# Forming the 32x32 inverses of three units by squaring on TensorE instead of column by column on VectorE

## The reference

```
for t in range(S):
    y[:, :, t] = einsum('bhd,bhde->bhe', rt, state)
    Sa = einsum('bhde,bhe->bhd', state, at)
    state = state * wt[:, :, None, :] - einsum('bhd,bhe->bhde', Sa, bt) + einsum('bhd,bhe->bhde', vt, kt)
h = x @ w_in;  x = maximum(0.01 * h, h) @ w_out            # 3072 x 320, 2048 wide
out = (sigmoid(x @ w_gate) * (x @ w_val)) @ w_out2          # 1536 wide
```

## Time and profile before

| what | value |
|---|---|
| time, median of 3 runs | 1166.05 us (1156.57 to 1169.82) |
| the profiled execution | 1176.43 us |
| its span, first to last instruction | 1174.7 us |
| TensorE busy | 1061.2 us, 90% |
| VectorE busy | 596.3 us, 51% |
| ScalarE busy | 397.6 us, 34% |
| mean granted TensorE clock | 0.956 of full |
| DMA queue of instructions (q8) | 125 packets, 2.05 MB |

### The profile page before, as it was taken

The page is one execution under the profiler, slowest core; times in us unless marked ns, Lnnn a source line. Parts: engine busy times, 40 slices in busy tenths (PEclk is TensorE's granted clock), DMA queues, the critical chain, the costliest instruction groups (busy, mean ns, idle before and its releaser), DMA issues.

```text
span 1174.7 us, 35939 instructions
## 1 busy us (share of the span) xinstructions
PE 1061.2 (90%) x15840; PEld 905.7 (77%) x15840; DVE 596.3 (51%) x1307; ACT 397.6 (34%) x782; POOL 109.4 (9%) x100
## 2 busy tenths in 40 slices
PE   3476595888999999989999999999999999999998
PEld 3476474776878787877778787888888888888887
DVE  8674674796667865666756232443323232322322
ACT  2323232333443533343344334553322222222322
POOL 7201102022020202020200000000000000000000
PEclk9996698988999998989999999999999999999999
DMA  5836215536353533444351205330010102020000
GB/s 174 260 70 217 57 29 142 130 93 172 85 139 87 165 84 107 114 131 94 105 140 51 70 8 170 102 93 23 15 45 1 59 1 59 1 59 1 23 1 23
DMA packets 134985, 99.79 MB, mean 85 GB/s; under 512 B 96560, under 2 KB 111920, under 8 KB 134832
## 3 DMA queue, kind: packets, MB, share of 16 engines
q1 hardware_dynamic: 132384, 85.06, 27.2%
q0 software_dynamic: 2448, 12.45, 3.0%
HBM read 78.61 MB, written 18.87 MB: 83 GB/s over the span
## 4 chain that ended last, share of the span: by engine, by line
PE 75%; DVE 9%; issue 8%; DMA 3%; ACT 2%; POOL 1%; SPq 1%; ACTq 0%; DVEq 0%; POOLq 0%
PE pair_low L866 12%; PE pair L919 11%; PE pair_low L919 6%; PE bank L919 6%; DVE prod L1402 3%; PE bank L939 3%; PE bank L938 3%; PE bank L937 3%; DVE t_unit L1406 2%; PE bank L840 2%; PE bank L831 2%; PE pair_low L883 2%; PE pair_low L884 1%; PE pair_low L885 1%; PE bank L883 1%
## 5 line engine op out<-in xcount | busy, mean ns | idle before, releaser
L1452 DVE TENSOR_TENSOR g_lo<-g_full,g_hi 128x512 fp32r<-128x512 f32 x168 | 122.7, 730 | 237.1 <-ACT g_hi L1167 237.0
L1167 ACT CAST g_hi<-g_full 128x512 fp32r<-128x512 f32 x168 | 104.4, 621 | 134.7 <-DVE g_full L1504 131.6
L866 PE MATMUL pair_low<-x_hi,w_up 128*128 128x512 f32 x440 | 131.8, 432 | 6.2 <-ACT x_hi L1176 3.4
L1160 ACT ACTIVATE g_full<-pair_low 128x512 f32<-128x512 f32 x88 | 52.7, 599 | 211.3 <-PE pair_low L866 198.6
L1402 DVE TENSOR_TENSOR prod<-t_unit,p_unit 128x126 f32<-128x126 f32 (+22 forms) x341 | 93.9, 275 | 24.8 <-DMA p_unit<-p_dram 14.6
L1406 DVE TENSOR_TENSOR t_unit<-t_unit,prod 128x126 f32<-128x126 f32 (+22 forms) x341 | 96.7, 284 | 11.7
L866 PEld LDWEIGHTS pair_low<-x_hi,w_up 128*128 128x128 f32 x440 | 82.3, 200 | 25.8 <-ACT x_hi L1176 3.5
L1504 DVE TENSOR_TENSOR g_full<-pair,h_sb 128x512 f32<-128x512 f32 x36 | 24.9, 691 | 112.8 <-PE pair L919 112.0
L866 PE MATMUL pair_low<-x_lo,w_up 128*128 128x512 f32 x264 | 78.4, 407 | 0.0
L1504 DVE TENSOR_TENSOR g_full<-bank,h_sb 128x512 f32<-128x512 f32 x36 | 24.9, 691 | 94.7 <-PE bank L919 86.3
L383 POOL TENSOR_TENSOR k_sb<-k_sb,inv 128x512 f32<-128x512 f32 x24 | 32.5, 1360 | 368.0 <-DMA k_sb<-in_kF 368.0
(11 more groups left out here) (232 smaller groups left out, 2564.4 us busy)
## 6 DMA issues: line engine op xcount, KB each, us to landing
b_sb<-in_bF SPq DMA_DIRECT2D x12, 512.0 KB, 6.3
a_sb<-in_aF SPq DMA_DIRECT2D x24, 256.0 KB, 6.4
k_sb<-in_kF SPq DMA_DIRECT2D x12, 512.0 KB, 5.0
v_sb<-in_vF SPq DMA_DIRECT2D x12, 512.0 KB, 6.7
r_sb<-in_rF SPq DMA_DIRECT2D x12, 512.0 KB, 8.6
p_unit<-p_dram SPq DMA_DIRECT2D x22, 256.0 KB, 4.1
w_raw<-in_wF SPq DMA_DIRECT2D x20, 260.0 KB, 3.6
stage<-in_w_out POOLq DMA_DIRECT2D x7, 640.0 KB, 7.2
```

The costliest lines, as they stand in the source:

```text
L866: last = nc.tensor.matmul(up_bank(m)[:], lhs, rhs, start=(e == 0), stop=(e == len(products) - 1))
L1160: nc.scalar.activation(g_full[:], up_bank(m)[:], ACT.Lrelu).then_inc(g_ready, 1)
L1167: nc.scalar.copy(g_hi[:, m % 2], g_full[:]).then_inc(g_hi_ready, 1)
L1452: nc.vector.tensor_tensor(g_lo[:, m % 2], g_full[:], g_hi[:, m % 2].bitcast(F32), ALU.subtract).then_inc(g_lo_ready, 1)
```

## The change

For units 0, 1 and 2 the inverse is formed on TensorE. With X the negated and masked scores of one 32x32 block (strictly triangular, so that its 32nd power is zero), T = (I + X)(I + X^2)(I + X^4)(I + X^8)(I + X^16). The kernel keeps powers X^(2^k) and their transposes, and a running product. Five levels k = 0 to 4 follow the scores. Each level multiplies, for 16 places j and four diagonal 32x32 blocks (groups) of the array, the transposed power with the power and the running product, and makes the next transposed power.

```diff
-            pe_a_ka(pe, 0, None)
-            pe_a_ka(pe, 1, None)
+            fill(pe, 30)
+            pe_scores(pe, 0, 0)
+            pe_scores(pe, 0, 1)
+            fill(pe, 4)
             pe_a_ka(pe, None, 0)
             pe_a_ka(pe, None, 1)
-            pe_a_ka(pe, 2, None)
-            pe_a_ka(pe, 3, None)
+            pe_level(pe, 0, 0)
             pe_kb(pe, 0)
+            pe_level(pe, 0, 1)
             pe_kb(pe, 1)
+            pe_level(pe, 0, 2)
...
+        def pe_scores(pe, u, c):
...
+            for q in range(TQ):
+                j = TQ * c + q
+                for i in range(2):
+                    b_t, a_t = b_sb[half(i, D), u % 2, c, q], a_sb[half(i, D), n % 5, q]
+                    for h in range(2):
+                        rows, tok = slice(L * i + C * h, L * i + C * h + C), slice(C * h, C * h + C)
+                        plain = nc.tensor.matmul(o_n[rows, j], b_t[:, tok], a_t[:, tok], start=True, stop=True)
+                        turned = nc.tensor.matmul(o_nt[rows, j], a_t[:, tok], b_t[:, tok], start=True, stop=True)
+                    cross = nc.tensor.matmul(o_cr[upper(i), j], b_t[:, 0:C], a_t[:, C:L], start=True, stop=True)
...
+        def pe_level(pe, u, k):
...
+            for j in range(2 * TQ):
+                for group in range(4):
+                    rows = rows_of(group)
+                    product = nc.tensor.matmul(o_x[rows, j], turned[rows, j], moving[rows, j], start=True, stop=True)
+                if k < 4:
+                    for group in range(4):
+                        rows = rows_of(group)
+                        square = nc.tensor.matmul(o_xt[rows, j], powers[rows, j, 0:C], turned[rows, j],
+                                                  start=True, stop=True)
...
+        def fill(pe, count):
+            for _ in range(count):
+                nc.tensor.matmul(bank[0][:, 0:P], ident[:], ident[:], start=True, stop=True)
...
+        def act_level(act, u, k):
...
+            nc.scalar.copy(powers_of(u)[:, :, 0:C], src).then_inc(bank_emptied[bank_of(f"x{k}", u)], 1)
+            bk = bank_of(f"xt{k}", u)
+            nc.scalar.copy(turned_of(u), bank[bk][:].rearrange("p (j t) -> p j t", t=C)
+                           ).then_inc(bank_emptied[bk], 1)
...
-        STEPS = {(2, 0): [0, 1, 2, 3, 4, 5, 6], (2, 1): [7], (2, 2): [], (2, 3): [8], (2, 4): [], (2, 5): [],
-                 (2, 6): [9], (2, 7): [], (3, 0): [10], (3, 1): [], (3, 2): [11], (3, 3): [], (3, 4): [12], (3, 5): [],
+        STEPS = {(2, 0): [0, 1, 2], (2, 1): [3], (2, 2): [4], (2, 3): [5], (2, 4): [6], (2, 5): [7], (2, 6): [8],
+                 (2, 7): [], (3, 0): [9], (3, 1): [10], (3, 2): [], (3, 3): [11], (3, 4): [12], (3, 5): [],
```

More of the change, by code:

```diff
@@ L423, in gpsimd_program @@
             pool_k(pool, 3)
[L424 to L428, removed]
+            pool_b(pool, 4)
+            pool_a(pool, 4)
+            pool_b(pool, 5)
+            pool_a(pool, 5)
+            load_piece(pool, 4)
+            load_piece(pool, 5)
             pool_k(pool, 4)
             pool_k(pool, 5)
+            load_piece(pool, 6)
+            load_piece(pool, 7)
             for n in range(6, 8):
@@ new lines, in act_masks, with act_cr @@
+        def act_masks(act):
+            act.wait_ge(constants_set, CONSTANTS)
+            for group in range(4):
+                rows, i, h = rows_of(group), group // 2, group % 2
+                nc.scalar.copy(eye[rows], ident[rows, rows])
+                last = nc.scalar.mul(minus_up[rows], mask[rows, C * h:C * h + C], -1.0)
+            last.then_inc(masks_set, 1)
+        def act_cr(act, u):
+            filled(act, "cr", u)
+            if u >= 2:
+                act.wait_ge(cross_multiplied, 2 * (u - 1))
+            src = bank[bank_of("cr", u)][:].rearrange("p (c q t) -> p c q t", c=2, t=C)
+            for i in range(2):
+                last = nc.scalar.mul(p_cross[upper(i), u % 2], src[upper(i)], -1.0)
+            last.then_inc(bank_emptied[bank_of("cr", u)], 1)
@@ new lines, in t_place, with act_t @@
+        def t_place(group):
+            rows, h = rows_of(group), group % 2
+            return t_sb[rows].rearrange("p c q t -> p (c q) t")[:, :, C * h:C * h + C]
+        def act_t(act, u):
+            filled(act, "x4", u)
+            multiplied(act, "u", 2 * u - 1)
+            src = bank[bank_of("x4", u)][:].rearrange("p (j t) -> p j t", t=C)
+            for i in range(2):
+                last = nc.scalar.copy(t_place(2 * i), src[upper(i)])
+            last.then_inc(t_upper, 1)
+        def act_t_unit(act, u):
+            if u == FORMED:
+                multiplied(act, "x4", FORMED - 1)
+            wait(act, t_stored, 32 * (u - FORMED))
+            wait(act, column_ready, (C - 1) * (u - FORMED))
+            nc.scalar.copy(t_unit.rearrange("p r t -> p (r t)"), restart[:, 1:2].to_broadcast([P, C // 2 * C])
@@ L1274, in scalar_start @@
             act_cross(act, 3)
-            act_kb(act, 2)
-            act_kb(act, 3)
+            for i in range(2):
+                split_hi(act, i)
             act_u(act, 2)
@@ L1280, in scalar_start @@
             act_ut(act, 3)
-            for i in range(4, 8):
-                split_hi(act, i)
+            act_kb(act, 2)
+            act_kb(act, 3)
+            split_hi(act, 2)
+            split_hi(act, 3)
+            act_cr(act, 2)
+            act_level(act, 2, 0)
+            split_hi(act, 4)
             act_kb(act, 4)
+            act_level(act, 2, 1)
             act_kb(act, 5)
+            split_hi(act, 5)
+            act_level(act, 2, 2)
+            split_hi(act, 6)
+            split_hi(act, 7)
+            act_t(act, 2)
             act_x(act, 0)
@@ L1357, in dve_constants @@
             nc.vector.memset(restart[:], 0.0).then_inc(vector_set, 1)
-            for tile in (pair_low, pair, bank2, bank3, bank6, bank7):
+            for tile in (pair_low, pair, pair_mid, bank6, bank7):
                 nc.vector.memset(tile[:], 0.0).then_inc(vector_set, 1)
@@ new lines, in dve_sum @@
+        def dve_sum(dve, u, k):
+            multiplied(dve, f"x{k}", u)
+            if k == 1:
+                dve.wait_ge(sum_begun, u + 1)
+            else:
+                dve.wait_ge(bank_emptied[3], turn(f"x{k - 1}", u, 1))
+            total = powers_of(u)[:, :, C:2 * C]
+            if k == 3:
+                multiplied(dve, "xt3", u)
+                bk = bank_of("xt3", u)
+                nc.vector.tensor_tensor(turned_of(u), blocks(bank[bk]), over_blocks(eye), ALU.add
+                                        ).then_inc(bank_emptied[bk], 1)
+                term, bk = blocks(bank[bank_of("x3", u)]), bank_of("x3", u)
+            else:
+                dve.wait_ge(bank_emptied[2], turn(f"x{k}", u, 0))
+                term, bk = pair_mid[:].rearrange("p k (j x) -> p (k j) x", x=2 * C)[:, :, C:2 * C], 3
+            nc.vector.tensor_tensor(total, total, term, ALU.add).then_inc(bank_emptied[bk], 1)
@@ L1525, in vector_start @@
             dve_y(dve, 1)
-            for i in range(4):
-                split_lo(dve, i)
+            dve_decay(dve, 5)
+            split_lo(dve, 0)
+            split_lo(dve, 1)
             dve_st(dve, 2)
@@ L1533, in vector_start @@
             dve_y(dve, 3)
-            dve_decay(dve, 6)
-            for i in range(4, 8):
-                split_lo(dve, i)
+            split_lo(dve, 2)
+            split_lo(dve, 3)
+            dve_power(dve, 2)
             dve_ka(dve, 4)
             dve_ka(dve, 5)
+            split_lo(dve, 4)
+            dve_sum(dve, 2, 1)
+            split_lo(dve, 5)
+            dve_sum(dve, 2, 2)
+            split_lo(dve, 6)
+            dve_sum(dve, 2, 3)
+            split_lo(dve, 7)
+            dve_t(dve, 2)
             dve_x(dve, 0)
+            dve_decay(dve, 6)
         def vector_first_steps(dve):
-            inverse_first(dve, 2)
-            inverse_columns(dve, 2, 0, 6)
             dve_g_low(dve, 0)
```

336 lines of the change are left out of this document (212 added, 124 removed), and 12 rows, old and new, of tables (START_BANKS, START_ORDER).

## The result

The changed kernel takes **1249.01 us**, the median of 4 runs (1246.57 to 1252.98); the kernel before takes 1165.04 in the same comparison (4 runs, 1156.57 to 1169.82). The ratio is 1.073, with an interval of 1.066 to 1.080: slower by 84 us. The forecast was 1250, in 1155 to 1280.

What follows compares the result with a forecast made beforehand. The prediction took instruction blocks arriving one after another to bound the new start stage: +99 there and -10 in g = 2 make 1265 on 1176.4, less 10.4 gives 1255, leaned to 1250 us, range 1155 to 1280.

Steps and rivals of the forecast that it cites:

- The mechanism and its count: Start stage: 6,469 pairs bring about 51 instruction packets; TensorE stands 1 to 2 us after every 126 pairs.
- The size of the block: Start stage: 42 instruction blocks at 4.2 us and 8 loaded ones at 6.1, ending near 240 us, +99 us.
- The cover: Levels of the start stage: copies out of PSUM hide under code loading and cost nothing; uncovered, 18 us.
- g = 2 and 3: After the start stage: shorter chain to `rhs(5)`, net -10 us, between -16 and 0.
- The clock: Start stage: starving invites TensorE's lower clock level, but blocks still execute within their loading time, so this moves little.
- 16 to 27 ns a pair: Start stage: execution price of a small-matmul pair, 2.1 to 3.4 us for 126 pairs, below a block's 4.0 us.
- Rival 1: Start stage: code is there in time, so the stage takes 138 us; median 1153 us; chance 27%.
- rival 3: Start stage near 150 us with blocks at about 2.7 us, gain given back, 1166 us within 1%; chance 6%.
- Rival 2: Start stage: code in time, but low clock and dear small tiles, 188 us; median 1203 us; chance 12%.
- the difference of profile and median: Whole kernel: the profiled execution was taken as 10.4 us above the median, so 1265 became 1255.
- leaning: Whole kernel: a small shift towards the 4.0 us block took the forecast from 1255 to 1250 us.

Runs made afterwards that it cites:

- Experiments 1 and 2: Changed kernel plus 632 independent, unread small matmuls in one dense row before unit 2's scores: 8 columns, 1292.00 us (one run); 32 columns, 1281.11 us, ratio 1.099.
- experiment 5: Changed kernel with the levels' powers, transposes and running product in bfloat16, one pair per matmul instead of two: 1211.32 us, 1.035 of the kernel before.
- experiment 6: Changed kernel with the MLP steps put back in their old places, seven in the first place of g = 2: 1257.31 us, 1.074 of the kernel before.
- experiments 1 to 3: The two dense-row runs on the changed kernel (1292.00, 1281.11 us), and the same 632 matmuls of 8 columns before `first(0)` in the kernel before: 1200.89 us, one run.

## Why the prediction was right

**The mechanism and its count.** The count of pairs held: 6,469 forecast, 6,468 matmuls and 6,469 weight loads in the trace. Packets in the stage: 50, forecast about 51. "TensorE stands 1 to 2 us after every 126 pairs" is what most of the ten stretches show (one stops for 0.9 us only, since it executes for 2.54, and one for 0.3, since it executes for 3.27). Experiments 1 and 2 give the block alone, without a dependence and whether the columns are 8 or 32; the times of the packets show what each stop waits for; experiment 5 gives time back at 3.4 us for each block of pairs taken out.

**The size of the block.** Forecast: 42 at 4.2 and 8 at 6.1 us, a mean of 4.5. Measured: 3.39 to 3.94 unloaded, 5.16 and 5.91 loaded. The blocks of the earlier trace rows were dearer, and I leaned only a little away from them. With 50 blocks from 17 us on, 214 us, the mean is 4.3: part of what the blocks gave back went to waits. So the first product came at 231.4 (and 237.0 in the twin of experiment 6) for 240, +90.6 for +99.

**The cover.** "The copies lie under the loading and I price them at nothing": no wait for ScalarE's copies is among the large ones. But VectorE's sums into the running product and its last copy into `t_sb` show (L1583, 3.9 us in three waits above, and L1591, 2.2 at `first`), and `v_nu` 3.9; about 10 us that I had at nothing. They and the shorter blocks cancel in part. One more stop is not the code's, though the profile writes "issue" at it: the last 3.96 us before the first product end 0.1 us after VectorE's last piece of `x_lo`, and in experiment 5 the same stop (4.2) bears the name of `x_lo`. The kernel before had it too (3.4), so it changes nothing in the sum.

**g = 2 and 3.** "-10 us, between -16 and 0". The traces show -20.5, but five kernels with the changed kernel's later code have a rest of 1011.7 to 1024.6 us, mean 1016.6, and two with the old one 1033.9 and 1030.8. So the gain is about 16 us, give or take 5 (my estimate from this spread), at the upper bound. `rhs(5)` starts 51.3 us after the first product; 49 was forecast and 65.4 it had been. The chain behind it, 231 to 283 us:

```profile
243.59 0.50 issue
244.09 0.59 ACT p_sb L1175
...
249.95 1.71 DMA p_dram<-p_sb
...
257.81 8.51 DMA w_raw<-in_wF
...
266.48 1.25 DVE decay L1533
...
278.18 0.69 DVE g_lo L1653
279.01 0.76 PE pair_low L963
```

`first(4)` no longer waits for `t_sb`, and the store and load of T are gone from SyncE's queue. How the 16 us divide between that and the steps' places is not settled; experiment 6 speaks against a large part for the steps, since with the old places the rest is 1020.2, within the spread of the five.

**The clock.** The stage's granted clock fell to 0.63 from 0.86, as I had thought. The unloaded stretches at 1.00 (3.39 and 3.79 us) and at 0.50 (3.59 to 3.94) hold as many pairs in nearly the same time, so it cost little here. One reading of mine has no row behind it: I put L753 of the earlier trace rows "at the slow clock", but the clock record of the kernel before begins at 74.6 us, and L753 ran at 62.8 to 64.9. The choice of 16 to 27 ns a pair loses a support by that; the stage's own figure is (153.2 - 9.1 of `fill`) / 6,400, or 22.5 ns of busy time a pair.

**The rivals.** Rival 1 (code in time, 138 us) and rival 3 need blocks of about 2.7 us or less; none of the stretches above is shorter than 3.39. Rival 2 (188 us) needs code that is in time and 27 ns of execution a pair; the levels' own stretch at 125.94 us executes in 1.93 us, 15 ns a pair, at the low clock, the stage's mean is 22.5, and TensorE stands idle for 78 of its 231 us, mostly for issue. The first 162 pairs of the scores ran in 1.81 us, 11 ns each, before the first starved stretch. The Trainium skill (Runtime: NRT & Kernel Launch, Instruction fetch mechanics) has block crossings as mostly hidden. The trace does not agree: 38 of the 50 packets of the start stage are followed by such a stop, for 0.3 to 2 us of 3.4 to 4 in the unloaded stretches, and in the pads of experiments 1 to 3 every block shows one.

**The sum.** +70 between the traces, +84 between the medians; I had +89 -10.4 for the difference of profile and median, less 5 of leaning. The forecast of 1250 hit 1249 by luck as well as by its steps. For the profiled execution it gives 1265, and 1246.62 came: the start stage was 8 us too long in it and the gain behind it 10 too small in this trace (6 by the mean of the five). Then 10.4 us went off for the difference of profile and median and 5 for leaning, and the first of these had the wrong sign here: the profiled execution after stood 2.4 below its median.

What stays open: what a packet waits behind under other transfers (experiments 1 and 2 have loaded stretches of 4.0, 5.1 and 7.3 us; in the longest the packet starts 4.4 us after the resumption and takes 1.43, but no run varies the load alone), how the rest's 16 us divide, and how many blocks can lie ready ahead of TensorE (222 pairs ran before the first stop, less than two blocks).

## What to carry to other kernels

Count the instructions of a dense stretch, not only its work: here 127 pairs of weight load and matmul in a dense row cost at least 3.4 us, or 27 ns a pair, however short they execute. A stage whose matmuls are shorter than that is bound by its own program text, and shows it as "issue" with no semaphore awaited, and with one packet of the instruction queue to each stop. Look at those packets: "issue" alone can also be a wait that the profile doesn't name, as at the first product here. An algorithm that trades 93 steps of another engine for 4,400 pairs of TensorE must find them a place between long matmuls (21 ns a pair here), or use a type that needs one pair in place of two. A thin DMA share and a thin busy share together don't mean that a stage waits for a dependence.

## What the runs showed of the hardware

- A dense row of independent 32x32 matmuls runs in a beat of 128 pairs, mostly 3.45 or 3.73 us long, nearly half of it idle, with the DMA engines 2% busy. Eight or 32 moving columns make no difference (1.89 and 1.93 us of execution).
- In that beat the packet of the instruction queue starts about 1.1 us after TensorE resumes and takes 0.9 to 1.4 us (experiments 1 and 2), and the next resumption comes about 1.4 us after its end (1.06 to 1.62 in 38 cases of the changed kernel).
- With the DMA engines 54 to 92% busy, stretches of 127 or 128 pairs took 4.0 to 7.3 us; the packet started up to 4.4 us after the resumption and took no more than 1.43.
- The pads execute in 1.24 us for 128 pairs at a granted clock of 0.96 and in 1.89 at 0.50.
- 24 small pairs set among 128x128 matmuls of 320 and 512 columns cost 0.51 us, of which 0.21 are the turns between tile shapes.
- Two executions of one start stage ended at 231.4 and 237.0 us; differences under some 6 us between single profiles of this kernel should not be trusted.
